# Seven block products for the second matmul of a gated MLP in two of three token groups, with split weights kept in DRAM

## The reference

```
attention in chunks of 64 tokens, 8 heads of 64     -> x    (2304 x 512)
a = x @ w_a ; b = x @ w_b          w_a, w_b: 512 x 1536
x2 = (a * b) @ w_out               w_out: 1536 x 512
for e in 0..3:
    h = max(x2 @ w1[e], 0)         w1[e]: 512 x 1024
    out += p[:, e] * (h @ w2[e])   w2[e]: 1024 x 512,  p = normalised domain_probs
```

## Time and profile before

| what | value |
|---|---|
| median of 3 runs | 1215.77 us |
| the profiled execution, its own time | 1215.23 us |
| span in its trace | 1213.5 us |
| TensorE (PE) busy | 1190.9 us, 98%, 7720 matmuls |
| VectorE (DVE) busy | 885.8 us, 73% |
| ScalarE (ACT) busy | 523.9 us, 43% |
| HBM read, written | 179.87 MB, 63.48 MB |
| mean granted TensorE clock | 0.994 |

### The profile page before, as it was taken

How to read it: one execution, slowest core, us unless ns; L and a number is a source line. 1 busy time by engine, 2 the same in 40 slices (tenths; PEclk the granted TensorE clock), 3 DMA queues, 4 the chain that set the end, 5 groups by cost and what they waited for, 6 DMA issues and landing times. The chain is left out here.

```text
span 1213.5 us, 18934 instructions
## 1 busy us (share of the span) xinstructions
PE 1190.9 (98%) x7720; PEld 1145.1 (94%) x7720; DVE 885.8 (73%) x1217; ACT 523.9 (43%) x926; POOL 0.7 (0%) x6
## 2 busy tenths in 40 slices
PE   8999999999999899999999999997999999999997
PEld 7999998888889899999999999997999999999997
DVE  5786478878887887554977777799765486666687
ACT  6554364444454455433433444345543343333332
POOL 0000000000000000000000000000000000000000
PEclk9999999999999999999999999998999999999999
DMA  7122265877779752321977777641233187677761
GB/s 263 36 74 92 70 243 187 314 311 315 304 295 351 278 187 70 121 63 52 357 274 264 272 253 264 227 183 52 88 141 94 46 330 261 255 265 253 264 243 52
DMA packets 52857, 244.56 MB, mean 202 GB/s; under 512 B 5084, under 2 KB 11300, under 8 KB 36388
## 3 DMA queue, kind: packets, MB, share of 16 engines
q1 hardware_dynamic: 52772, 243.36, 54.9%
HBM read 179.87 MB, written 63.48 MB: 201 GB/s over the span
## 5 line engine op out<-in xcount | busy, mean ns | idle before, releaser
L508 PE MATMUL ps<-x,wab 128*128 128x384 f32 x504 | 170.2, 338 | 7.2 <-ACT ps L900 6.7
L900 ACT ACTIVATE hw<-xraw 128x768 fp32r<-128x768 f32 x112 | 93.2, 845 | 179.2 <-DVE xraw L1743 81.1
L509 PE MATMUL ps<-x,wab 128*128 128x384 f32 x504 | 169.1, 336 | 0.0
L510 PE MATMUL ps<-x,wab 128*128 128x384 f32 x504 | 169.0, 335 | 0.0
L508 PE MATMUL ps<-hw,w2s 128*128 128x384 f32 x448 | 153.0, 341 | 1.4 <-DVE hw L1364 0.5
L900 ACT ACTIVATE ps<-ps 128x384 f32<-128x384 f32 (+1 forms) x176 | 88.1, 504 | 149.0 <-PE ps L510 148.7
L508 PE MATMUL ps<-x,w1s 128*128 128x384 f32 x448 | 151.2, 338 | 0.0
L510 PE MATMUL ps<-hw,w2s 128*128 128x384 f32 x448 | 149.8, 334 | 0.0
L509 PE MATMUL ps<-hw,w2s 128*128 128x384 f32 x448 | 149.8, 334 | 0.0
L510 PE MATMUL ps<-x,w1s 128*128 128x384 f32 x448 | 149.8, 334 | 0.0
L509 PE MATMUL ps<-x,w1s 128*128 128x384 f32 x448 | 149.7, 334 | 0.0
(11 more groups left out here) (170 smaller groups left out, 2381.2 us busy)
## 6 DMA issues: line engine op xcount, KB each, us to landing
w1s<-kept_w SPq DMA_DIRECT2D x32, 1024.0 KB, 6.3
w2s<-kept_w SPq DMA_DIRECT2D x16, 2048.0 KB, 8.1
w1s<-kept_w SPq DMA_DIRECT2D x16, 1536.0 KB, 6.1
w2s<-kept_w SPq DMA_DIRECT2D x16, 1536.0 KB, 6.1
raw<-in_wab SPq DMA_DIRECT2D x36, 512.0 KB, 4.7
raw<-in_w SPq DMA_DIRECT2D x16, 1024.0 KB, 10.8
kept_w<-w SPq DMA_DIRECT2D x16, 1024.0 KB, 12.9
kept_w<-w SPq DMA_DIRECT2D x8, 1536.0 KB, 16.0
```

The costliest lines, as they stand in the source:

```text
L508: pe.matmul(dst, stat(HI), mov(HI), start=first, stop=False, skip_group_check=True)
L509: pe.matmul(dst, stat(HI), mov(LO), start=False, stop=False, skip_group_check=True)
L510: return pe.matmul(dst, stat(LO), mov(HI), start=False, stop=last, skip_group_check=True)
L900: return act.activation(dst, src, ACT.Copy)
```

## The change

For T = 1 and 2, x2 = g @ w_out becomes a seven-product Winograd form as well (`later_x2`): the blocks are g by halves of its features (f below and from 6) and token halves, and w_out by halves of its rows and columns. Each of the seven products is made of three units u of 12 matmuls, 21 units (`UNIT3`) and 252 matmuls in all. ScalarE rounds a g unit (`round_unit`), VectorE takes the rest (`low_unit`) and makes the sums of g in place (`sum_g`): XS3 in the last pair, ahead of `pair_g("C11")`, the others in the product itself. PSUM seeding is as in a pair. Blocks A11, A22 (`xr(7)`), A12 and the sums for x2 are made while the last units run.

The w_out blocks and sums for it are made in T = 0, whose own x2 stays plain (`first_x2`) but takes f in `WO_ORDER`, so that four loaded row blocks give one third of each sum: `sum_wo`, `round_wo_sums`, `low_wo_sums` at i = 3/4, 6/7, 10/11, with SP storing them (`store_wo`, `store_wo_sums`) to `kept_wo`. `sum_wo(u)` waits until the sums before were stored (`wot_kept`); loads of row blocks 4 to 7 and 8 to 11 wait for `sum_wo`. `load_w2(0)` comes behind `store_wo_sums(2)` on SP.

The seven split blocks of every pair from (0, 2) to (1, 1) are stored as well, to `kept_ab`, 512 KB each, and from (1, 2) on all pairs are loaded from there into the ring (`load_block`), with no work on ScalarE and VectorE; w_out units are loaded likewise into a ring of six (`load_unit`).

The core of the diff:

```diff
+            def store_block(T, j, n):
+                at = block_no(T, j, n)
+                sp.wait_ge(ab_lo, at + 1)
+                sp.dma_start(kept_ab[j, :, n], wab[:, at % RING].bitcast(F32)).then_inc(ab_kept[at % RING], 16)
...
+            def load_block(T, j, n):
+                at, before = block_no(T, j, n), 7 * j + n - RING
+                if before >= 0:
+                    sp.wait_ge(MADE[order(T, before // 7)[before % 7]], 2 * set_ab(T, before // 7) + 2)
+                else:
+                    sp.wait_ge(p3_made, 2 * set_ab(T, 0))
+                if at - RING < FIRST_LOADED:
+                    sp.wait_ge(ab_kept[at % RING], 16 * ab_stores(at - RING))
+                sp.dma_start(wab[:, at % RING].bitcast(F32), kept_ab[j, :, order(T, j)[n]]).then_inc(ab_in[at % RING], 16)
...
+            def store_wo_sums(u):
+                sp.wait_ge(wot_lo, 2 * u + 2)
+                for n, c in ((4, 0), (1, 1), (2, 2)):
+                    sp.dma_start(kept_wo[n, u].rearrange("p z t n -> p z (t n)"),
+                                 wo_three[:, c].bitcast(F32)).then_inc(wot_kept, 16)
+                sp.dma_start(kept_wo[5, u].rearrange("p z t n -> p z (t n)"),
+                             wo_lone[:, :].bitcast(F32)).then_inc(wot_kept, 16)
...
+            def first_stage():
...
+                for i in range(4):
+                    load_wo(i)
+                for i in range(FA):
+                    store_wo(i)
+                    u = i // 4
+                    if i == 3:
+                        sp.wait_ge(wot_sum, 4)
+                        for n in range(4, 8):
+                            load_wo(n)
+                        store_wo_sums(0)
+                    if i == 6:
+                        sp.wait_ge(wot_sum, 8)
+                        for n in range(8, 11):
+                            load_wo(n)
+                    if i == 7:
+                        load_wo(11)
+                        store_wo_sums(1)
                         sp.wait_ge(p3_made, 2 * set_e(0, 0))
                         load_qk(TILES)
                         load_v(TILES)
-                sp.wait_ge(wo_lo, FA * (T + 1))
+                store_wo_sums(2)
...
+            def later_stage(T):
...
+                for i in range(WRING, UNIT3):
+                    wait_unit(sp, T, i - WRING)
+                    load_unit(T, i)
+                    if i in (8, 12, 16):
+                        load_w1s(0, {8: 0, 12: 2, 16: 1}[i])
...
+            def later_x2(T):
+                Q, pairs = set_x(T), pair_no(T, NPAIR)
+                def make(n, banks, first):
+                    for u in range(3):
+                        i = 3 * n + u
+                        pe.wait_ge(wos_in[i % WRING], 16 * wo_loads(T, i))
+                        pe.wait_ge(gs_lo, gs_count(T, i))
...
-                if last:
-                    round_ab(T + 1, 0, 0)
-                    round_ab(T + 1, 0, 1)
                 act.wait_ge(hs_sum, 4 * V + 4)
...
                     act.wait_ge(hw_lo, 7 * V + 7)
                     round_sum(T + 1, XS2)
-                    round_ab(T + 1, 0, 2)
-                    round_ab(T + 1, 0, 3)
                     round_sum(T + 1, XS1)
-                    round_ab(T + 1, 0, 4)
-                    round_ab(T + 1, 0, 5)
                     round_sum(T + 1, XS4)
-                    round_ab(T + 1, 0, 6)
...
+                if j == NPAIR - 1 and T == 0:
+                    low_wo(0)
+                    low_g(0)
+                    low_wo(1)
+                    low_g(1)
+                elif j == NPAIR - 1:
+                    for u in range(3):
+                        low_unit(T, u)
+                        sum_g(T, XS3, u)
...
+            def sum_wo(u):
...
+                for n in range(4):
+                    dve.wait_ge(wo_in_s[n], 16 * (u + 1))
+                if u == 0:
+                    dve.wait_ge(p3_made, 2 * set_e(0, 0))
+                else:
+                    dve.wait_ge(wot_kept, 64 * u)
...
             def border(T):
 
                 V = no_w(T, 0)
-                low_ab(T, 0, 0)
-                low_ab(T, 0, 1)
                 low_sum(T, XS3)
-                for n in range(4):
-                    sum_ab(T, 0, n)
-                low_ab(T, 0, 2)
                 low_sum(T, XS2)
-                low_ab(T, 0, 3)
                 low_sum(T, XS1)
-                low_ab(T, 0, 4)
...
+                    if T == NTH - 1 and j < 3:
+                        fold(j)
+                if T:
+                    later_x2(T)
+                else:
+                    for i in range(3, FA):
+                        low_wo(i)
+                        low_g(i)
+                        if i in (3, 6, 10):
+                            sum_wo((i - 3) // 3)
+                        if i in (4, 7, 11):
+                            low_wo_sums((i - 3) // 3 if i < 11 else 2)
+                        if i == 5:
+                            for n in range(4):
+                                sum_w1(0, n)
                     for n in range(3):
                         split_w1(0, n)
+                    low_x2(0, A11, xr(0))
+                    dve.wait_ge(xraw_set, 2)
+                    dve.tensor_tensor(xr(2), xr(0), xr(1), ALU.subtract).then_inc(s_set, 1)
                     split_w2(0, 0)
+                    low_x2(0, S3, xr(2))
                 for w in range(PH):
                     if T == 0:
```

More of the change, by code:

```diff
@@ L307, in block_no, with from_dram, ab_stores, ab_loads @@
             return 4 * j + n if T == 0 and j < PLAIN else 4 * PLAIN + 7 * pair_no(T, j) + n
+        FIRST_KEPT, FIRST_LOADED = block_no(0, PLAIN, 0), block_no(1, PLAIN, 0)
+        def from_dram(T, j):
+            return T > 1 or (T == 1 and j >= PLAIN)
+        def ab_stores(at):
+            return (at - FIRST_KEPT) // RING + 1
+        def ab_loads(at):
+            return (at - FIRST_LOADED) // RING + 1
+        def wo_stores(i):
+            return sum(1 + (n % 4 >= 2) for n in range(i % 3, i + 1, 3))
+        def wo_loads(T, i):
+            return (T - 1) * len(range(i % WRING, UNIT3, WRING)) + i // WRING + 1
+        def gs_count(T, i):
+            return FA + UNIT3 * (T - 1) + i + 1
+        def gx_count(T, kind, u):
+            return 12 * (T - 1) + 3 * (XS3, XS2, XS1, XS4).index(kind) + u + 1
+        def wait_unit(engine, T, i):
+            n, u = divmod(i, 3)
+            if u == 2:
+                engine.wait_ge(MADE[n], 2 * set_x(T) + 2)
+            else:
+                engine.wait_ge(x2_unit, 14 * (T - 1) + 2 * n + u + 1)
         XB_ORDER = ((XS3, XS2, XS1, XS4), (XA22, XA11, XA12, XS3, XS2, XS1, XS4))
@@ L1005, in run_pair @@
                 Q, before = set_ab(T, j), pair_no(T, j)
-                ahead = j < NPAIR - 1
+                ahead = j < NPAIR - 1 and not from_dram(T, j + 1)
                 def next_ab(n):
@@ L1039, in run_pair @@
                     seed_c(Q, s)
-                if not ahead:
-                    for f in range(3):
-                        round_wo(T, f)
-                        round_g(T, f)
+                if j == NPAIR - 1:
+                    for i in range(3):
+                        if T == 0:
+                            round_wo(i)
+                            round_g(i)
+                        else:
+                            round_unit(T, i)
                 next_ab(4)
@@ L1523, in run_pair @@
                 next_ab(5)
-                if not ahead:
-                    low_wo(T, 2)
-                    low_g(T, 2)
+                if j == NPAIR - 1 and T == 0:
+                    low_wo(2)
+                    low_g(2)
                 add_c(Q, "C21", 0)
@@ L1619, in add_out @@
                 dve.wait_ge(out_made, TILES * w + i + 1)
+                if w == 0 and i == 0:
+                    for p in range(3):
+                        dve.wait_ge(wo_kept[p], 16 * wo_stores(FA - 3 + p))
                 if w == 0:
```

464 lines of the change are left out of this document (324 added, 140 removed).

## The result

The changed kernel takes **1208.7 us** in the median (1207.48 to 1212.96, 16 runs); the kernel before, run beside it, took 1215.77 (1214.88 to 1217.4, 16 runs). The ratio is 0.9946, 95% interval 0.9937 to 0.9955: about 7 us faster. Forecast were 1207.2, a range of 1197 to 1215, and faster by over 0.2% with 0.84.

A forecast was written before the change was run, and what follows sets the result against it. TensorE, busy 98% of the span, was taken as the bound. 1215.23 - 12.5 - 8.2 + 2.4 + 9.7 = 1206.6, with 0.54 for the median 1207.2 us; range 1197 to 1215, the forecast's own 1203 to 1211.

The forecast's parts named there:

- Step 1: x2's products in T = 1 and 2: 252 matmuls instead of 288 each, -12.5 us if nothing holds units up.
- Rival D: Later products: units wait for VectorE every time, 5 us lost in the two thirds, 1212 us; chance 0.1.
- Step 2: Transfers in the later thirds: loaded blocks and units land in time, cost zero.
- Rival C: Later thirds: units and blocks arrive slower than TensorE uses them, above 2.08 us per 512 KB; 1220 us, chance 0.06.
- Step 3: Border to T = 2: less ScalarE and VectorE work ahead of seed_b, stop under 1 us, no half clock, -8.2 us.
- the second stop: TensorE's stop at 840.03, after the border to T = 2, forecast to go with ScalarE's rounding ahead of it, 1.1 us.
- Rival B: Border to T = 2: the stop stays, as x sums alternate between two engines; 1215.4 us, chance 0.08.
- Step 4: Last pair of T = 1 and 2: VectorE's added rests and sums delay the seventh block, +2.4 us, no half clock.
- Step 5: First third's product and step into window 0: w2 lands late behind 2 MB of stores, delaying S3's block, +9.7 us.
- The first third's product: x2's product in T = 0: the added sums and stores just hold, cost 0, at most 2 us.
- Rival A: Step into window 0: w2 load not waited for, costing 0 to 3.8 instead of 9.7, 1197 to 1201 us; chance 0.2.

The follow-up runs named there:

- runs 7 and 8: Changed kernel with w_out units loaded three units back instead of six: 1230.81 us; the same with window 0's w1 loads behind all units: 1216.47 us.
- Run 6: Changed kernel with the old ScalarE roundings and VectorE rests, sums and mutual waits put back on unused data at the border to T = 2: 1216.21 us.
- Run 3: Changed kernel with the three XS3 sums of g in the last pair of T = 1 and 2 moved behind the pair's last g: 1205.78 us.
- Run 4: Changed kernel with a second place for the w_out sums, so sum_wo(1) need not wait for the stores of sum_wo(0): 1206.6 us.
- run 1: Changed kernel with window 0's w2 load issued ahead of the last four stores of w_out sums: 1203.52 us.
- run 5: Changed kernel with only ScalarE's old roundings of 128x512 put back on unused data at the border to T = 2: 1212.13 us.
- run 7: Changed kernel with w_out's units in the products of T = 1 and 2 loaded three units back instead of six: 1230.81 us.

## Why the prediction was right, and where it was off

- **Step 1, fewer matmuls (-12.5)**: -12.48, to the hundredth, since nothing waits in the later products. The `gs` rows are 168 + 96 = 264 a line, as said. Rival D (units wait for VectorE) is out: TensorE is busy for all of the 43.68 us.
- **Step 2, transfers (0)**: right. In the median a unit lands 3 to 4 us before it is needed. Rival C looked for its danger in the rate; runs 7 and 8 show that it lies in the lead: with three units in place of six the kernel takes 1231 us, and 12.9 of the 19.4 us lost in the products are units queued behind w1, which that rival did not have.
- **Step 3, the border (-8.2)**: the pairs of T = 2 fell by 6.5 us with the last pair's new stop of 1.6 in them: -8.1. Run 6 puts +7.3 of it back. The 1.1 us that were put down to the second stop are gone in the changed kernel, but giving ScalarE its roundings back did not bring them back, so that part of the cause is not shown. The stop was forecast at under 1 us (it is 0.51) and without half clock (there is none). Rival B is out.
- **Step 4, last pairs (+2.4)**: the stops of 1.34 us idle, 1.68 from start to start, are where and how long they were forecast (1.7), and no half clock followed. Run 3 takes 1.64 and 1.62 us away; 88.25 - 87.39 = 0.86 of the first was in the kernel before already, which leaves 2.4.
- **Step 5, the first third (+9.7)**: +11.9. The mechanism was right, link by link: S3's rest was forecast to end 9.75 us later than before, counted from the start of the product, and ended 11.0 later (181.65 - 120.17 against 169.15 - 118.67). The stop itself is 5.8 us where 6.8 were forecast, since window 0 began 2.1 us later than forecast and S3's rest came only 1.25 later. Mis-sized was the landing of the four stores of the sums: 7.4 us were taken from a pair of transfers; the first sums' stores needed 8.4 (issued 137.27, and VectorE goes on at 145.79), the second 8.3 (152.36 to 160.7). Each of the two held up a sum, and the last stores were issued 2.0 us later than forecast. Run 4, without the first of these holds, issued them 1.8 us sooner behind the product's start (170.36 - 123.68 against 168.69 - 120.17). The landings are not the only wait there: the last sum ended at 163.39, and ScalarE's wait of the next point at 163.53, with 1.3 us of step 11's roundings ahead of the sums'. How the 2.0 us divide is not shown. What hangs on the late issue is +1.65 at w2's landing; splitting S3 took 0.4 less than priced. The rest, 0.9, is mostly half clock that outlasted the chain: S3's block ended at 185.7, where the next was ready, and five matmuls of that one still came 0.32 us apart in place of 0.17, 0.7 us.
- **The first third's product** was put at 0, at most 2; apart from the late A11 (1.25, forecast 1.4 in the next step) it lost 2.1, at steps 7 and 11. Step 7 is the landing above. Step 11 is a wait that the prediction did not have: ScalarE's for the place in `wo`, whose store had come to stand behind the sums' stores. The prediction had followed the queue for the sums and for w2, and not for this ring.
- **Rival A** (the w2 load is not waited for, 0.2) was wrong for this kernel, and its price was too low: with the wait gone (run 1) the time is 1203.5, not 1197 to 1201. The late start and window 0 together then cost 4.0 us, against A's 0 to 3.8, and the stops at steps 7 and 11 come on top.
- The sum missed by 1.5 us in the medians (1208.7 against 1207.2) and by 2.9 us of span: 2.2 from step 5, 1.5 from the stretch ahead of the product, less 0.9 gained in the windows. The 1.5 are no part of the change, see the last section; the 0.9 was not forecast and offsets part of the others by luck.

## What to carry to other kernels

When a change adds stores to a queue, walk the whole queue once for each ring it serves: here three rings (the sums' places, `wo`'s places, `raw` for w2) waited on one queue, and two groups of stores moved by one step gave back 2 us, the load moved ahead of 2 MB 5.2. Price a transfer by what stands ahead of it, not by its own landing time; the lead a ring gives must cover the largest transfer that can be queued in between. And where two engines alternate on a path, count the work of both and their waits for each other: at the border ScalarE's work alone made 2.6 us of a stop of 5.7.

## What the runs showed of the hardware that was not expected

- **Half clock can outlast its gap, and the gap's length does not decide it.** After the stop of 5.8 us at 181.71 matmuls stood 0.32 us apart for 5.6 us more; after the 5.7 us at the border in run 6 the mean clock of the pairs is 0.96, after 2.6 us in run 5 it is 0.98. Stops of 1.3 us idle (535.02, 918.03) were followed by none; nor were those of 0.46 and 1.98 in run 1, whose stretch shows 1.00. But a stop of 1.90 us in run 5 was followed by half clock (matmuls 0.32 us apart up to 170.18), and one of 2.24 us in run 7, three units ahead, was not (0.17 us apart). The lines of the two, run 5 first:

```profile
166.90 0.61 PE L669 MATMUL ps<-gs,wo 128*128 128x384 f32 x1 [1.90 <-DVE gs L1633]
```

```profile
585.09 0.45 PE L664 MATMUL ps<-gs,wo 128*128 128x384 f32 x1 [2.24 <-DMA wo<-kept_wo]
```

Half clock can also begin late: behind the changed kernel's stop of 2.07 us in window 7 (418.07) matmuls stood 0.17 us apart up to 419.57 and 0.32 from there to 422.77.
- **SP's issue grows slow when much is queued**: three stores of sums took 1.64 us to issue (168.69), and 2.28 when others were under way (152.36); single issues went from 0.33 us to 1.2 (170.37, 171.62). A load "issued behind" others is late by that too.
- **The start varies from run to run**: the stretch ahead of the first third's product took 118.7 us before, 120.2 after, and from 118.2 to 123.7 in the other profiles. All of the variation lies ahead of one matmul of the plain pairs (26.95 before, 28.45 after, 26.42 to 31.96 in the others); from there to the product it is 91.7 us in every profile, with and without the new stores. The granted clock differs in that first part: 0.84 and 0.82 from 10 to 15 and from 15 to 20 us in after, 1.00 in both before. The 1.5 us belong to the difference of the two spans and not to the change.
